# Three edits in a fused attention, soft-MoE and FFN kernel: the slots' softmax, the loads of w and u, and the first load of v

## What is computed

```python
# 1. linear attention with decay: B, H, S, D = 4, 8, 768, 48
for t in range(S):
    kt, vt, rt = (k[:, :, t], v[:, :, t], r[:, :, t])
    cur = np.einsum('bhd,bhe->bhde', u[None] * kt, vt)
    y[:, :, t] = np.einsum('bhd,bhde->bhe', rt, state + cur)
    state = w[None, :, :, None] * state + np.einsum('bhd,bhe->bhde', kt, vt)
# 2. soft MoE over x = y as 3072 x 384, with phi 384 x 32 (8 experts, 4 slots each)
logits = x @ phi
d = np.exp(logits - logits.max(0, keepdims=True))
d /= d.sum(0, keepdims=True) + 1e-09          # over the tokens: the slots' softmax
slot_input = d.T @ x
# each expert: np.maximum(slot_input[e] @ w1[e], 0.0) @ w2[e]
c = np.exp(logits - logits.max(1, keepdims=True))
c /= c.sum(1, keepdims=True) + 1e-09          # over the slots: the rows' softmax
x = c @ slot_out
# 3. FFN with ELU: 384 -> 2048 -> 384
h = x @ w_in
out = np.where(h > 0.0, h, np.exp(np.minimum(h, 0.0)) - 1.0) @ w_out
```

## Time and profile before

| | |
|---|---|
| runs | 393.88, 393.62, 391.74 us; median 393.62 |
| the profiled execution | 392.18 us, of which the span shown by the trace is 390.4 |
| PE busy | 374.2 us, 96% of the span |
| DVE, ACT, POOL busy | 69%, 56%, 26% |
| DMA | 51.80 MB in 87,280 packets, 77,776 of them under 512 B |
| granted TensorE clock | 1.00 over the span |

### The profile page before, as it was taken

One profiled execution on the slowest core, in us unless ns is written; L12 is line 12 of the kernel. 1 busy time (PEld: TensorE's weight loads), 2 busy tenths in 40 slices (PEclk: granted clock), 3 DMA queues, 4 the chain that ended last, 5 costly groups with the idle time before them and its releaser, 6 DMA issues.

```text
span 390.4 us, 11439 instructions
## 1 busy us (share of the span) xinstructions
PE 374.2 (96%) x4373; PEld 333.0 (85%) x4373; DVE 267.6 (69%) x512; ACT 219.6 (56%) x498; POOL 103.3 (26%) x136
## 2 busy tenths in 40 slices
PE   6898999999889999999999999999999999999996
PEld 3787898989775454589999999999999999999996
DVE  4787788778767620699867767667777667776671
ACT  2896778777772131588564446444644464455441
POOL 7797777777640000355200000000000000000000
PEclk9999999999999999999999999999999999999999
DMA  7989899999999999920020002000200020002002
GB/s 152 254 151 186 199 234 233 227 255 254 235 303 426 430 432 403 373 64 2 0 83 1 2 0 81 0 0 0 81 0 0 0 81 0 0 0 82 2 2 81
DMA packets 87280, 51.80 MB, mean 133 GB/s; under 512 B 77776, under 2 KB 83024, under 8 KB 85200
## 3 DMA queue, kind: packets, MB, share of 16 engines
q1 hardware_dynamic: 82368, 50.21, 43.1%
q10 hardware_dynamic: 4880, 1.16, 1.4%
HBM read 45.86 MB, written 4.72 MB: 130 GB/s over the span
## 4 chain that ended last, share of the span: by engine, by line
PE 79%; DMA 10%; SPq 3%; issue 3%; ACT 3%; DVE 1%; POOL 1%; DVEq 0%; POOLq 0%; ACTq 0%
PE psum L976 17%; PE psum L978 17%; PE psum L977 17%; PE psum L911 6%; DMA w_out_raw<-in_moe_w_out_dram 4%; PE psum L603 4%; DMA r_raw<-in_r_dram 3%; PE psum L643 3%; PE psum L826 3%; PE psum L686 3%; PE psum L667 2%; PE psum L656 2%; PE psum L696 2%; DMA v_sb<-in_v_dram 1%; PE psum L703 1%
## 5 line engine op out<-in xcount | busy, mean ns | idle before, releaser
L978 PE MATMUL psum<-w_out_hi,elu_lo 128*128 128x384 f32 x372 | 125.8, 338 | 0.0
L976 PE MATMUL psum<-w_out_hi,elu_hi 128*128 128x384 f32 x372 | 125.7, 338 | 0.0
L977 PE MATMUL psum<-w_out_lo,elu_hi 128*128 128x384 f32 x372 | 125.3, 337 | 0.0
L1405 ACT ACTIVATE exp_h<-psum 128x512 f32<-128x512 f32 x96 | 57.6, 600 | 97.3 <-PE psum L911 97.0
L1246 DVE SCALAR_TENSOR_TENSOR elu<-psum,neg_part 128x512 f32<-128x512 f32 x96 | 66.3, 690 | 57.1 <-ACT neg_part L1392 57.1
L977 PEld LDWEIGHTS psum<-w_out_lo,elu_hi 128*128 128x128 f32 x372 | 69.8, 188 | 3.9
L976 PEld LDWEIGHTS psum<-w_out_hi,elu_hi 128*128 128x128 f32 x372 | 70.4, 189 | 0.0
L978 PEld LDWEIGHTS psum<-w_out_hi,elu_lo 128*128 128x128 f32 x372 | 69.9, 188 | 0.0
L1238 DVE TENSOR_TENSOR elu_lo<-elu,elu_hi 128x512 fp32r<-128x512 f32 x96 | 66.3, 691 | 0.6
L1280 ACT ACTIVATE scores<-ident_wide,bonus 128x128 f32<-128x128 f32 x192 | 58.8, 390 | 5.0 <-DVE bonus L1028 4.9
L1392 ACT ACTIVATE neg_part<-exp_h 128x512 f32<-128x512 f32 x96 | 60.0, 626 | 1.7 <-DVE elu L1246 1.3
(11 more groups left out here) (155 smaller groups left out, 403.6 us busy)
## 6 DMA issues: line engine op xcount, KB each, us to landing
w<-in_moe_w_dram SPq DMA_DIRECT2D x8, 1536.0 KB, 13.6
w_sb<-in_moe_w_dram SPq DMA_DIRECT2D x8, 1024.0 KB, 6.3
out_dram<-out_sb SPq DMA_DIRECT2D x24, 192.0 KB, 1.9
w_sb<-in_moe_w_dram SPq DMA_DIRECT2D x8, 512.0 KB, 6.2
w_out_raw<-in_moe_w_out_dram SPq DMA_DIRECT2D x4, 768.0 KB, 15.7
r_raw<-in_r_dram SPq DMA_DIRECT2D x12, 192.0 KB, 3.2
r_raw<-in_r_dram SPq DMA_DIRECT2D x24, 96.0 KB, 3.4
w_in_sb<-in_moe_w_in_dram SPq DMA_DIRECT2D x1, 2304.0 KB, 19.4
```

The lines of the kernel that those rows point to most:

```text
L976: pe.matmul(acc, hi, w_out_hi[:, f, :], start=(f == 0), stop=False)
L977: pe.matmul(acc, hi, w_out_lo[:, f, :], start=False, stop=False)
L978: m = pe.matmul(acc, lo, w_out_hi[:, f, :], start=False, stop=(f == KF2 - 1))
L1405: act.activation(exp_h[:, f % 2, :], banks[4 + f % RING][:, :], ACT.Exp).then_inc(exp_done, 1)
```

## The change

Three parts.

1. **The loads of the head.** w is loaded as 8 rows (each twice, for both halves of a pair) into a corner of `tables_T`; PE turns it into PSUM twice, once for DVE and once for ACT. u is loaded as one row into partition 0 and PE spreads it to 128 partitions with a matmul by ones; ACT copies it to `u_row`, and POOL waits for that copy (`u_ready`). PE's four fills are split: two ahead of these, two behind.
2. **The first v.** Its three DMAs are issued by SP behind the first r, not by ACT behind the table swap.
3. **The slots' softmax.** The exponentials of the last chunk come straight from `logits_now`, are turned right behind the maxima, and slot_in(3) is put ahead of the matmul that spreads the maxima. ACT scales the early slots ahead of the exponential of `fold_w`; DVE multiplies `fold_w` by `fold` between `den_cols` and `slot_parts`. The last chunk's logits, and the inverses of the early rows' sums, move behind `slot_T`.

```diff
@@ names of steps
-        (D_TOP_ROW, D_FOLD_SHIFT, D_FOLD, D_DENCOLS, D_SLOT_PARTS, D_DENEPS, D_DENINV, D_SLOT_T,
+        (D_TOP_ROW, D_FOLD_SHIFT, D_DENCOLS, D_FOLD, D_SLOT_PARTS, D_DENEPS, D_DENINV, D_SLOT_T,
-        A_RESCALE, A_FOLD, A_EARLY_SLOTS, A_IDENT_R = range(1, 5)
+        A_RESCALE, A_EARLY_SLOTS, A_FOLD, A_IDENT_R = range(1, 5)
+        w_nat, u_nat = tables_T[0:H, 0, 0, :], u_row[0:1, :, :].rearrange("p h d -> p (h d)")
+        ps_w, ps_u = (banks[4][:, 0:H], banks[0][:, 0:H]), banks[1][:, 0:DM]
@@ SP
             sp.wait_ge(cleared, 1)
-            for half in range(2):
-                sp.dma_start(wcol[half * HP:half * HP + D, :], w_cols, allow_slow_non_contiguous=True
-                             ).then_inc(w_loaded, 16)
+            sp.dma_start(w_nat.rearrange("h (two d) -> h two d", two=2)[:, :, 0:D], w.unsqueeze(1).broadcast_to([H, 2, D])).then_inc(w_loaded, 16)
             load_r(0, 0)
+            load_v(0, 0)
             sp.wait_ge(k_loaded[0], LOADED)
@@ POOL
-            pool.wait_ge(u_loaded, 16)
+            pool.wait_ge(u_ready, 1)
@@ PE, the head
-            for i, n in ((2, 4), (3, 4), (6, 2), (5, 2)):
+            def fill(i, n):
                 pe.matmul(banks[i][:, 0:n * P].rearrange("p (n t) -> p n t", n=n), ones[:, :],
                           ones[:, :].unsqueeze(1).broadcast_to([P, n, P]), start=True, stop=True)
+            fill(2, 4)
+            fill(6, 2)
+            pe.wait_ge(const_set, 5)
+            pe.wait_ge(w_loaded, 16)
+            for at in ps_w:
+                pe.transpose(at, w_nat, ident[0:H, 0:H]).then_inc(w_turned, 1)
+            pe.wait_ge(u_loaded, 16)
+            pe.matmul(ps_u, ones[0:1, :], u_nat, start=True, stop=True).then_inc(u_spread, 1)
+            fill(3, 4)
+            fill(5, 2)
@@ PE, the slots
             pe.transpose(banks[0][0:1, 0:P], neg_top[:, 1:2], ident[:, :]).then_inc(pe_step, 1)
-            chunk_logits(CHUNKS - 1)
+            pe.wait_ge(exp_T_ready, 2)
+            pe.transpose(banks[1][:, P:2 * P], exp_T[:, :], ident[:, :]).then_inc(exp_turned, 1)
             slot_in(2)
+            slot_in(3).then_inc(x_used, 1)
             pe.wait_ge(dve_step, D_TOP_ROW)
             pe.matmul(banks[0][:, P:P + SLOTS], ones[0:1, :], top_row[0:1, :], start=True, stop=True
                       ).then_inc(pe_step, 1)
-            pe.wait_ge(exp_T_ready, 2)
-            pe.transpose(banks[1][:, P:2 * P], exp_T[:, :], ident[:, :]).then_inc(exp_turned, 1)
-            slot_in(3).then_inc(x_used, 1)
             slot_in(4).then_inc(early_slots_done, 1)
             slot_in(5).then_inc(pe_step, 1)
+            chunk_logits(CHUNKS - 1)
             keep_clock_up(2)
-            pe.wait_ge(dve_step, D_DENCOLS)
+            pe.wait_ge(dve_step, D_FOLD)
@@ DVE
-            dve.wait_ge(w_loaded, 32)
+            dve.wait_ge(w_turned, 2)
...
-            dve.wait_ge(act_step, A_FOLD)
-            dve.tensor_tensor(fold_w[:, 1, :], fold_w[:, 1, :], fold[:, :], ALU.mult).then_inc(dve_step, 1)
-            row_inverses(EARLY)
             dve.tensor_tensor(den_cols[:, :], slot_early[:, DM:DM + 1].broadcast_to([P, P]),
                               banks[3][:, DM:DM + 1].broadcast_to([P, P]), ALU.add).then_inc(dve_step, 1)
+            dve.wait_ge(act_step, A_FOLD)
+            dve.tensor_tensor(fold_w[:, 1, :], fold_w[:, 1, :], fold[:, :], ALU.mult).then_inc(dve_step, 1)
             dve.tensor_tensor(slot_parts[:, :, :], *(x[:, 0:DM].rearrange("p (q c) -> p c q", c=KD) for x in (slot_early, banks[3])),
...
+            logits_to_sbuf(CHUNKS - 1)
+            row_inverses(EARLY)
             row_weights(EARLY)
@@ ACT
+            act.dma_start(u_nat, u_flat).then_inc(u_loaded, 16)
             load(act, k_raw, k_dram, 0, 0, k_loaded)
             act.wait_ge(const_set, 5)
             act.activation(exp_warm[:, :], ident[:, 0:1], ACT.Exp)
-            act.dma_start(u_row[:, :, :].rearrange("p h d -> p (h d)"), u_flat.broadcast_to([P, DM])).then_inc(u_loaded, 16)
-            act.wait_ge(w_loaded, 32)
-            for rows, cols in w_halves:
+            act.wait_ge(w_turned, 2)
+            for rows, cols in w_halves_too:
                 m = act.copy(wpow[rows, 0, 0, :].rearrange("p (rev e) -> p rev e", rev=2), cols)
             m.then_inc(w_copied, 1)
+            act.wait_ge(u_spread, 1)
+            act.copy(u_row[:, :, :].rearrange("p h d -> p (h d)"), ps_u).then_inc(u_ready, 1)
...
-            load(act, v_sb, v_dram, 0, 0, v_loaded)
...
-            act.activation(exp_T[:, :], logits_T[:, CHUNKS - 1, :], ACT.Exp, bias=neg_top[:, 1:2]).then_inc(exp_T_ready, 1)
+            act.activation(exp_T[:, :], logits_now[:, :], ACT.Exp, bias=neg_top[:, 1:2]).then_inc(exp_T_ready, 1)
```

35 lines of the change are left out of this document (19 added, 16 removed).

## The result

| | before | after |
|---|---|---|
| median of 20 runs | 393.71 us (391.56 to 395.65) | 394.82 us (391.79 to 401.1) |
| profiled execution (span) | 392.18 (390.4) | 393.54 (391.8) |
| ratio after to before | | 1.0052, 95% interval 1.0032 to 1.0073 |

A forecast was written before the change was run, and what follows sets the result against it. PE (96% busy), nearly full attention engines and a byte-bound stretch at 144 to 161 us bound it; head 2.5 - 0.28 - 0.94 = +1.3, softmax -0.1, so +1.2 on 392.86: 394.1 us, range 391.0 to 396.6.

The forecast's parts named there:

- The meeting: In the head, POOL's four products of 1.0 us start amid DVE's table of decay powers; the two take turns.
- the anchor: End of DVE's k_nat of unit 1 in the head, 12.10 us in before; predicted +1.3 us.
- table's start: DVE's first reciprocal in the head, at 4.9 us against 4.50, as w's turn waits behind two PE fills.
- steps held by products: One to three of DVE's table steps in the head last 1.0 us more, standing still until POOL's product ends.
- POOL's first product: POOL's u*k in the head can begin at about 6.4 us (bounds 6.1 and 6.9), against 7.55 in before.
- wait for k_table falls away: Between r_pair and k_nat of unit 1, DVE's 0.28 us wait for PE's k_table goes: -0.28.
- k_nat not held: DVE's L1084, k_nat of unit 1, takes 0.42 us and not 1.36, POOL's products being over: -0.94.
- the third rival: POOL takes one more turn among DVE's table steps: a further 1.0 us, +2.2 and more, 395.1 to 396; chance 0.18.
- The softmax: In the slots' softmax, slot_parts starts 0.1 us sooner (bounds -0.3 and +0.1); counted as 0 to -0.1.
- w_out's landing still ends the experts' stretch: In the experts' stretch after the slots' softmax, the bytes of w_out's load set the end, as in before.
- Rival 4: DMA engines absorb the head's delay in units from 60 us; at most a third; nothing arrives: chance 0.05, 392.9 us.
- Costed at nothing: Head effects given no cost: the earlier r, v issued by SP, phi's four DMAs on ACT ahead of the table swap.

The follow-up runs named there:

- pool_waits: The changed kernel with one wait added: POOL starts its first product only once DVE has finished the table of powers; 393.98 us, ratio to before 1.0055.
- copy_as_max: The changed kernel with DVE's 128x4 table copy written as a two-operand maximum, memsets left in place; 395.08 us, ratio to before 1.0046.
- memsets_first: The changed kernel with POOL's three memsets of pads put ahead of the selects that build fold; 394.14 us, ratio to before 1.0033.
- pads_and_pool_waits: The changed kernel with POOL's pad memsets ahead of fold's selects and POOL's first product waiting for DVE's table; 392.74 us, ratio to before 1.0015.
- v_only: The kernel before with only the first v issued by SP instead of ACT; 393.50 us, ratio to before 1.0040.
- before_again: The kernel before, unchanged, measured again as if it were an experiment; 392.96 us, ratio to before 1.0012.
- before_pads_first: The kernel before with only POOL's three memsets of pads moved ahead of fold's selects; 393.47 us, ratio to before 0.9998.
- head_only: The kernel before with only the loads of w and u changed, v and slots' softmax as before; 394.83 us, ratio to before 1.0077.
- softmax_only: The kernel before with only the slots' softmax changed; 393.47 us, ratio to before 1.0043.

## Why the prediction was right, point by point

**The meeting** (DVE's table steps and POOL's products taking turns): right, and shown by the table of pool_waits. So were its place, its sign at the anchor, and that L1084 is no longer held (0.55 us at L1102).

**The size of the head** was off: +2.0 at the anchor for the +1.3 of the sum. Term by term, all from the rows above:

| term | predicted | measured |
|---|---|---|
| table's start | 4.9, +0.4 | 5.10, +0.6 |
| copy held by memsets | not seen | +0.5 |
| steps held by products | three at 1.0 us, ahead of L1014 | four at 0.74 to 0.80 us, 3.1 us in all |
| POOL's first product | 6.4 (6.1 to 6.9) | 7.13 |
| r_pair of unit 0 | 11.2, +2.5 | 11.89, +3.2 |
| wait for k_table falls away | -0.28 | -0.40 (1.66 us for 2.06 from r_pair to k_nat) |
| k_nat not held | -0.94 | -0.81 |
| anchor | 13.4, +1.3 | 14.10, +2.0 |

The terms that were mis-sized are the two ahead of the meeting: the table's start (0.2 us more than predicted) and the copy's hold (0.5, not seen). Together they are the 0.7 by which r_pair is late. The turns themselves came out at their sum by luck: three at 1.0 us were predicted and four at less than 0.8 measured, 3.0 against 3.1. The order was wrong. The two steps L1021 and L1024 passed in one gap, where the sum gave POOL a turn between them. And the steps from L1031 on are no gapless series: POOL slipped in between the two of L1031 and ahead of L1039.

POOL's start, 7.13 and not 6.4, is outside its bounds. The matmul that spreads u ran at the low rate, 1.62 us where the sum had 0.9 and 0.2 for the drain. It changed little, because the table was 0.7 later than predicted too, so that the first product met the step that the sum has it meet. Where one of the two moved alone, the turns changed: in copy_as_max the table was 0.5 ahead with POOL's start at 7.14, and three steps were held. By the number of turns the outcome is the third rival, one more turn and +2.2 at the anchor; by the reason for the 0.7 it isn't. That rival's mark, the last table step ending after 12, was missed by 0.15.

**The softmax**: -0.13 where -0.1 was predicted.

**What the experts' stretch does with it.** The prediction let bytes set its end and w_out's landing with it, and allowed an absorption of a third at most. PE's first matmul with w_out, in before and in after:

```profile
162.69 0.34 PE L959 MATMUL psum<-w_out_hi,elu_hi 128*128 128x384 f32 x1
```

```profile
164.16 0.34 PE L976 MATMUL psum<-w_out_hi,elu_hi 128*128 128x384 f32 x1
```

From the last copy of logits_now to there before took 162.69 - 120.50 = 42.19 us, and after 164.16 - 122.98 = 41.18, as did memsets_first, copy_as_max and pads_and_pool_waits (41.18 each). In before w_out's DMA ends the chain of this stretch; in after it is PE's and DVE's own steps. So of the 2.48 us by which after reached the softmax late (2.0 from the head, the rest lost on the way), 1.0 did not arrive, 0.13 of it the softmax's gain, and +1.4 in the span is left.

That a late softmax is absorbed by the load isn't shown by this pair. v_only reached it when before did (120.44) and took 41.33 us, without a wait for w_out on its chain, and before_again, at 121.76, 41.32. before_pads_first, at 121.78, took 42.01, and head_only, at 120.66, 41.81. So the 0.9 us that the execution of before lost to w_out came and went with the execution, and the sign "w_out's landing still ends the experts' stretch" failed. Rival 4 named an absorption by the DMA engines, but in the units of the attention, where after kept its 1.9 us up to unit 15.

**Costed at nothing**: v, rightly in the head (v_only moved the anchor by 0.06), open behind it. The earlier r, rightly: it was turned at 9.19, before the table was done. phi on ACT, rightly in after (the swap at 8.66 was only needed at 10.70), and not in general, as pads_and_pool_waits showed.

**The total**: 394.1 predicted, 394.82 measured. The sum had +1.2 on a level of 392.86 for before; the medians differ by 1.1 on a level of 393.71. So the error of 0.7 in the time is that of the level, taken from four executions. In the two profiled executions the difference is 1.4: a head too cheap by 0.7 and 0.5 lost on the way to the softmax, against 0.9 that before lost to w_out and after didn't. That +1.2 came as near as it did is luck in good part.

**Left open.** How much of the measured 0.3 to 0.5% is the head's meeting: in the one group that has both, head_only, which meets, and pool_waits, which doesn't, are 0.85 us apart, less than their intervals. How often the kernel before meets: one of four traces is all that says it. And how the medians of v_only and softmax_only came to stand 1.7 us above before in their group; before itself read 391.81, 393.24 and 394.11 on the chips of the three groups and 393.71 beside after, so the level moves by more than the intervals within one suggest.

## What to carry to other kernels

Before moving a GpSimd stretch earlier, or a VectorE chain later, lay both on one time axis: where two independent chains passed each other by 0.02 us, a change of 0.4 us in either cost about 0.8 us for each step held, and the unchanged kernel paid it too in one of four traces. A profiled execution is one throw; profile the unchanged kernel twice before an effect of one wait is read out of it. And a step that hides behind a hold is not free: with the hold gone, ACT's swap was the bound of the table.
